# A Fourier filter and an eight-expert layer on one core: zero stores, table loads, casts and the last inverse in another order

## The reference, cut to what matters

```python
def _attn_ref(x, filt_r, filt_i):            # x: 8 x 3072 x 256
    X = np.fft.rfft(x, axis=1)
    Y = X * (filt_r + 1j * filt_i)[None]
    return np.fft.irfft(Y, n=x.shape[1], axis=1)

def _moe_ref(x, w_gate, w1, w2, capacity):   # x: 24576 rows of 256, 8 experts, F = 1024
    N, D = x.shape
    logits = x @ w_gate
    expert_idx = np.argmax(logits, axis=1)
    # gate_w: the softmax probability of the chosen expert
    # rows go to their expert in order of index, at most 768 each; later ones are dropped
    h = np.maximum(np.einsum('ecd,edf->ecf', disp, w1), 0.0)
    y = np.einsum('ecf,efd->ecd', h, w2)
    # out[i] = gate_w[i] * y[expert, place] for kept rows, 0 for all others
```

## Time and profile before

| | us |
|---|---|
| median of 3 runs | 518.39 |
| lowest and highest | 517.58, 519.9 |
| the profiled execution | 520.91 |
| its span in the profile | 519.0 |

### The profile page before, as it was taken

The page is one execution under the profiler, slowest core; times in us unless marked ns, Lnnn a source line. Parts: engine busy times, 40 slices in busy tenths (PEclk is TensorE's granted clock), DMA queues, the critical chain, the costliest instruction groups (busy, mean ns, idle before and its releaser), DMA issues.

```text
span 519.0 us, 12606 instructions
## 1 busy us (share of the span) xinstructions
PE 472.5 (91%) x5432; PEld 428.4 (83%) x5432; DVE 243.5 (47%) x381; ACT 231.8 (45%) x434; POOL 182.2 (35%) x158
## 2 busy tenths in 40 slices
PE   5888999999999786399889999999999999999994
PEld 5767887588875472399889989999999999999993
DVE  1195538893499951478155303334432453134200
ACT  3634566555665465062154523434452454433320
POOL 0000000000000060053457788644877556684222
PEclk9999999999999999599899998999999999999997
DMA  8990000850017599900413159631199320681001
GB/s 291 412 370 7 1 3 3 282 209 3 3 44 228 213 373 378 337 3 21 143 42 121 52 168 403 219 124 53 39 383 357 90 86 32 230 336 45 32 33 35
DMA packets 37169, 80.47 MB, mean 155 GB/s; under 512 B 4944, under 2 KB 13808, under 8 KB 36592
## 3 DMA queue, kind: packets, MB, share of 16 engines
q1 hardware_dynamic: 30832, 66.92, 35.7%
q0 software_dynamic: 6272, 12.65, 7.2%
HBM read 40.20 MB, written 39.35 MB: 153 GB/s over the span
## 4 chain that ended last, share of the span: by engine, by line
PE 76%; issue 5%; DMA 5%; DVE 4%; SPq 4%; POOL 3%; ACT 1%; POOLq 0%; DVEq 0%; ACTq 0%
PE psum L1194 24%; PE psum L1208 22%; PE psum L435 7%; PE psum L422 6%; PE psum L452 4%; PE psum L406 4%; SPq L373 4%; DMA w_raw<-in_w 4%; PE psum L510 3%; PE psum L476 2%; DVE prod L726 2%; PE psum L579 2%; PE psum L466 1%; POOL o_gate L1098 1%; POOL out L1114 1%
## 5 line engine op out<-in xcount | busy, mean ns | idle before, releaser
L1023 DVE SCALAR_TENSOR_TENSOR hl<-psum,hh 128x384 fp32r<-128x384 f32 x128 | 69.7, 556 | 151.1 <-ACT hh L974 151.1
L1208 PE MATMUL psum<-w2h,hh 128*128 128x256 f32 x384 | 110.5, 288 | 0.0
L1208 PE MATMUL psum<-w2l,hh 128*128 128x256 f32 x384 | 109.2, 284 | 0.0
L1208 PE MATMUL psum<-w2h,hl 128*128 128x256 f32 x384 | 109.1, 284 | 0.0
L1194 PE MATMUL psum<-xh,w1h 128*128 128x384 f32 x256 | 87.5, 342 | 15.1 <-DVE xl L764 11.8
L974 ACT ACTIVATE hh<-psum 128x384 fp32r<-128x384 f32 x128 | 61.9, 492 | 75.1 <-PE psum L1194 74.9
L1194 PE MATMUL psum<-xl,w1h 128*128 128x384 f32 x256 | 87.0, 340 | 0.0
L1194 PE MATMUL psum<-xh,w1l 128*128 128x384 f32 x256 | 86.8, 339 | 0.0
L726 DVE TENSOR_TENSOR prod<-psum,fab 128x1024 f32<-128x1024 f32 x48 | 56.5, 1219 | 53.7 <-PE psum L406 42.6
L1114 POOL DMA_INDIRECT out<-o_out,token x48 | 50.6, 1054 | 85.6 <-ACT o_out L983 66.7
L1208 PEld LDWEIGHTS psum<-w2l,hh 128*128 128x128 f32 x384 | 74.3, 194 | 0.0
(11 more groups left out here) (107 smaller groups left out, 596.3 us busy)
## 6 DMA issues: line engine op xcount, KB each, us to landing
out<-zero SPq DMA_DIRECT2D x24, 1024.0 KB, 15.1
w_raw<-in_w SPq DMA_DIRECT2D x14, 1024.0 KB, 5.7
x_in<-in_x SPq DMA_DIRECT2D x18, 512.0 KB, 8.0
y_rows<-y SPq DMA_DIRECT2D x12, 512.0 KB, 4.5
fab<-in_fab SPq DMA_DIRECT2D x4, 1024.0 KB, 13.3
first_raw<-in_w SPq DMA_DIRECT2D x2, 1024.0 KB, 9.2
wbi<-in_wbi SPq DMA_DIRECT2D x4, 384.0 KB, 15.5
y_rows<-y SPq DMA_DIRECT2D x6, 256.0 KB, 9.0
```

The lines of the kernel that those rows point to most:

```text
L1023: nc.vector.scalar_tensor_tensor(out=hl[:, b % 2, f, :], in0=ps[(2, 3, 6, 7)[f % 4]][:, 0:TOK], scalar=0.0, in1=hh[:, b % 2, f, :].bitcast ...
L1208: mm = nc.tensor.matmul(ps[4 + (b * ST + s) % 2][:, 0:D], hx[:, b % 2, f, s * P:(s + 1) * P], wt[k][:, f, :], start=(f == 0 and m == 0), s ...
```

## The change

- The nine zero stores move on SP from the end of `sp_last_stage` to the end of `sp_last`, behind the loads of expert 1 and the row stores.
- At the start, tables 2 and 3 are loaded ahead of the second batch instead of behind it.
- In `pe_stage` the table of the stage's tokens moves in the last group from ahead of the inverse of group 6 to behind it; in the expert part it moves from behind down(0,2) to ahead of it.
- At a stage's end the inverse of group 7 comes ahead of all four turns of the next stage; ScalarE's list follows.
- ScalarE's two casts of expert 0 move one group up, from groups 6 and 7 to 5 and 6.
- VectorE makes expert 1's `w2l` after the route's last steps and the tokens instead of before them.

```diff
@@ sp_last_stage, sp_last
-            if r == 0:
-                sp.wait_ge(zero_set, 1)
-                sp.nop(nofuse=True)
-                for k in range(FIRST_ZEROS):
-                    sp.dma_start(out_z[k], zero_view).then_inc(first_zeroed, 16)

         def sp_last(sp, t, r):
             raw_load(sp, r, 1, 0)
             raw_load(sp, r, 1, 1)
             for c in range(products(t) // 2):
                 y_store(sp, t, c)
+            if r == 0:
+                sp.wait_ge(zero_set, 1)
+                sp.nop(nofuse=True)
+                for k in range(FIRST_ZEROS):
+                    sp.dma_start(out_z[k], zero_view).then_inc(first_zeroed, 16)
@@ pe_stage
-                    if h == NG - 1:
-                        pe_table(pe, tok, 7)
                     for i in turned_at(h):
...
                     if h == RANK_STEP:
                         pe_rank(pe, tok, 7)
+                    if h == NG - 1:
+                        pe_table(pe, tok, 7)
...
-            if a is not None:
-                pe_turn_z(pe, a, 0, r)
-                pe_turn_z(pe, a, 1, r)
             pe_inverse(pe, t, NG - 1)
             if a is not None:
-                pe_turn_z(pe, a, 2, r)
-                pe_turn_z(pe, a, 3, r)
+                for g in range(ZB):
+                    pe_turn_z(pe, a, g, r)
@@ act_stage
+                if t == last - 1 and h == NG - 3:
+                    act_split(act, r, 0, 0)
                 if t == last - 1 and h == NG - 2:
-                    act_split(act, r, 0, 0)
-                if t == last - 1 and h == NG - 1:
                     act.wait_ge(b_done, t * NG + NG - 2)
                     act_split(act, r, 0, 1)
-            if a is not None:
-                act_turned_z(act, a, 0)
-                act_turned_z(act, a, 1)
             act_back(act, t, NG - 1)
             if a is not None:
-                act_turned_z(act, a, 2)
-                act_turned_z(act, a, 3)
+                for g in range(ZB):
+                    act_turned_z(act, a, g)
@@ dve_experts
-                low_split(dve, r, 1, 1)
                 route(HOT, ROUTE_STEPS)
                 both()
+                low_split(dve, r, 1, 1)
                 turned(2)
@@ pe_experts
-            downs(0)
+            down(0, 0)
+            down(0, 1)
             if r == 0:

                 pe.wait_ge(hl_done, 2 * FT)
                 pe_table(pe, last - 1, 7)
+            down(0, 2)
             down(1, 0)
@@ sync, run
-                load_tables(sp, 0)
-                load_tables(sp, 1)
+                for g in range(4):
+                    load_tables(sp, g)
                 for c in range(NCH):
                     x_load(sp, first + 1, c, first)
-                load_tables(sp, 2)
-                load_tables(sp, 3)
```

10 lines of the change are left out of this document (5 added, 5 removed).

## The result

| | kernel before | changed kernel |
|---|---|---|
| median of 4 runs each, side by side on one chip, us | 517.99 | 510.67 |
| lowest and highest | 516.22, 519.9 | 509.57, 511.71 |
| the profiled execution | 520.91 | 511.06 |
| its span | 519.0 | 509.2 |
| TensorE matmuls busy | 472.5 (91%) | 474.1 (93%) |

The ratio is 0.9858, with a 95% interval of 0.9816 to 0.99: 7.3 us faster, where 12.9 were forecast. The predicted 505.5 is 5.2 us too low, and the time lies 0.7 above the upper end of the range, 510.0.

What follows compares the result with a forecast made beforehand. TensorE, 91% busy, was taken as the bound, with its idle stretches and slow clock recoverable. Terms -11.8 - 1.9 + 3.5 - 1.4 - 0.2 - 1.1 = -12.9 us, applied to the 518.39 median, gave 505.5; range 501.5 to 510.

Steps and rivals of the forecast that it cites:

- part 3: Expert part, table ahead of down(0,2) and w2l later: +1.8 to 1.9 us at turn(2) alone, masked while zeros end late.
- part 4: Stage ends, last inverse ahead of the turns hides TensorE's wait for t_in: -0.7 us each, -1.4 in all.
- part 5: End of stage 2, table behind inverse(6) and earlier casts: -0.2 us; stop in the logits gone: -1.1; neither bounded above 0.
- late instruction fetch: Last logits of stage 2: TensorE's 1.16 us stop taken for a fetch that freed DMA engines would spare, -1.1 us.
- GpSimd's chain: From zeros' end at 229.6 through output sends and block 2's gather to turn(2) at 240.8; cost with late zeros +3.5 us.
- no cost taken: Row stores before ScalarE's relu in up(0): landing put at 3 to 4 us within some 4 us of slack, cost 0.
- (a): Zeros end before 228, so the table's order sets turn(2): +1.9 us in place of +3.5, 503.9; chance 0.2.
- (b): Zeros take 31 us or more: +3.4 us more, 508.9; chance 0.12.
- (c): Row stores land late beside the zeros, TensorE stops some 5 us at up(0)'s fifth group: 510.6; chance 0.08.
- (d): Instruction-fetch stalls move under the zeros, beside up(0) and up(1): up to 3.1 us, 508.6; chance 0.04.
- (e): Slower than before: GpSimd's wait for zeros at turn(2) eats the gain, zeros ending from 245: 521; chance 0.03.
- (f): Expert-1 load leaves early but a gather or gate row holds the start: total as before, 518; chance 0.03.

Runs made afterwards that it cites:

- part 1 alone: Kernel before with only the nine zero stores moved behind the row stores: 517.65 against 524.81 us, ratio 0.9849.
- parts 3 and 4 undone: Two kernels, each the changed kernel with one order restored: expert table and w2l, ratio 0.9823; turns ahead of the last inverse, 0.9886.
- part 5 undone: Changed kernel with stage table again ahead of inverse(6) and ScalarE's expert-0 casts a group later, run twice: ratios 0.9862 and 0.9849.
- all together: Changed kernel with zeros one by one, row-store wait late, old expert and stage table orders and cast places, run twice: ratios 0.9711 and 0.9722.
- zeros early with part 3 undone: Changed kernel with zeros in one burst behind the constants and the old order of expert table and w2l: 509.97 us, ratio 0.9799.
- part 6 undone: Changed kernel with the second x again ahead of tables 2 and 3: 517.22 us, ratio 0.9827.
- late-relu experiment: Changed kernel with ScalarE's wait for the row stores moved from the first relu to its first write of o_out: 516.67 us, ratio 0.9842.

## Why the prediction was wrong, step by step

**Right.** The loads leave at 182 (181.7), up(0) waits for nothing and runs at full clock, the two stops of 0.68 go, and so does the one in the last logits. (The prediction has the loads land before 195 at 14.3 us from 183.3; that sum gives 197.6, still ahead of the 199.27 that it needs.) turn(2) follows up(1) by 28.9, within the 28 to 32 named. The zeros bind: in the ten profiles of kernels that have them behind the rows (the changed one three times, and those with one part undone or done alone), turn(2) comes 39.3 to 40.1 us after the first zero's issue, whatever stands between, although up(1) moves against the zeros by 2 us. In the kernels without zeros there it is up(1) that sets it, 27.6 to 28.0 us later with the table ahead of down(0,2) and 26.0 to 26.3 with the old order. The masking of part 3 and its price alone (1.4 to 2.0 measured, 1.8 to 1.9 forecast) are thereby shown. So is what part 4 gives at the stage ends (0.8 and 0.8 measured, 0.7 each forecast).

**Mis-sized, up to up(2).** The sum gave -12.9 there; the two profiles have -10.1 (258.93 to 248.81). The constant just named splits the difference of 2.8, since only two terms lead to turn(2) when the zeros bind.

**When the zeros start: 203.6, not 202.0, 1.6 late.** The step that failed is part 5, its "-0.2" and "-1.1" with nothing above 0 as the worst case. TensorE's rank matmuls start only 1.4 us earlier than before (202.72 against 204.13), not 2.7; the last 0.3 is SP, which has to issue the last rows first. At the last forward step of stage 2 TensorE is still 2.5 us ahead (173.12 against 175.58), more than part 4's 1.4: part 4 gave 1.7, and 0.8 is luck, since the stops at 33 and 40 us happened to be shorter. From there to the rank matmuls the changed kernel takes 29.60 us and the kernel before 28.55. So this stretch, where part 5 was to gain 1.3, lost 1.05. The 1.41 for `hot_hi` went, but a stop of 1.17 us came up inside the table instead, 0.85 ahead of inverse(7), and half clock behind them:

```profile
175.84 0.30 PE L533 MATMUL psum<-hot_hi,hot_lo 128*128 128x96 bf16 x3
177.31 1.05 PE L533 MATMUL psum<-hot_hi,hot_lo 128*128 128x96 bf16 x21 [1.17 <-issue]
179.22 2.39 PE L422 MATMUL psum<-wbi,prod 64*64 64x96 f32 x64 [0.85 <-DVE prod L728]
182.57 4.76 PE L466 MATMUL psum<-v_in,wgs 128*32 128x128 f32 x96 [0.96 <-ACT v_in L623]
```

The same stretch, from the start of the last forward step of stage 2 to that of the rank matmuls, in all eighteen profiles:

| us | profiles |
|---|---|
| 26.84, 26.85 | zeros early, zeros one by one |
| 28.55 | kernel before |
| 28.75 to 28.82 | part 1 alone; parts 3 and 4 undone; part 5 undone, first; zeros left out; all together, both times |
| 29.59, 29.60 | changed kernel, first two; zeros early with part 3 undone |
| 30.28 | changed kernel, third |
| 32.45 to 34.51 | kernel before once more; part 5 undone, second; part 6 undone; row-store wait moved |

In all sixteen profiles with the zeros moved the stop of 1.16 us is gone from the logits, so that much of "moving zeros also frees the DMA engines around 185 us" came. But in most of them the time is lost again some microseconds later, in a stop in the last turns or in half clock. The table's place itself is worth 0.14 us where no half clock follows (logits to logits 51.99 against 52.13). Part 5 as a whole shows in no median: 518.63 undone against 517.79.

The stop in the table is not the stop of the earlier trace rows moved. It stands after the same 3 matmuls of the table in all eleven profiles with part 5's order, and that of the earlier trace rows after the same 42 logits in both profiles of the kernel before. In the list of the changed kernel these two places are 21 + 64 + 42 = 127 matmuls apart. The two early stops, at 33 to 35 and at 39 to 41 us, are 127 matmuls apart as well, at the same places in all eighteen profiles. With a weight load for each matmul that makes 254 instructions, near the 256 that the prediction cites for a block. So the prediction's late instruction fetch is well supported, though no row shows a fetch. In the old order the wait of 1.41 us for `hot_hi` stands some 2 us ahead of the earlier of the two places, and no stop shows there. That this wait hides it fits, and is not shown. Whether the stop needs full DMA engines is open too. The share is 0.18 in the stretch of the stop itself (columns as above), but they had been nearly full until 176:

```profile
176.00:177.30 1.30, 0.14 (x3) 0.04 (x1) 1.30 (x2) 0.84 (x2) 0.00 (x0) 1.00 0.18 56
```

The Trainium skill ("Runtime: NRT & Kernel Launch", Instruction fetch mechanics) calls such fetches mostly hidden; here stops of 0.2 to 2.4 us without any semaphore stand in every profile, two of them always at the same places, so the trace agrees only in part.

**The zeros' length and GpSimd's chain: 40.0 us from the first issue to turn(2), not 38.8.** The zeros took 29.1 us at 356 GB/s in all, not 27.6 at 360. At 356 GB/s, 29.1 us are 10.4 MB, and the sum had 9.9: the rate costs 0.3 and the bytes 1.2. The likeliest source of the 0.4 MB more is the load of expert 2's w1, issued right behind the zeros at 221.98; no run took it away, so this stays open. GpSimd's chain is 10.9, not 11.2.

**Wrong, but without effect.** The row stores were put at "no cost taken", and up(0) does stop at its fifth group (0.71 us), which the prediction had named as a sign of being wrong. They cost 2.1 us between up(0) and up(1) (11.49 against 9.35 with the row-store wait moved; the forecast had 9.1), more than half of it ahead of up(1), which the prediction did not see: the late relu delays VectorE's low halves, behind which `xl` of block 1 is made, at 213.53 to 214.54. The estimate of 3 to 4 us for landing was right (3.6 to 4.6); what was wrong was the slack. The last rows are ready at 202.37, but SP needs until 203.51 to issue their last two stores. ScalarE's four delayed relus come in one row of 1.64 us, and the low half then comes another 0.6 us later. The late-relu experiment shows the cost and that it is hidden, since the zeros bind: 2.1 us gained at up(1), none at turn(2).

**Wrong: from the profiled execution to the median.** The profiles differ by 9.8 us and the medians by 7.3. The prediction took its sum against one execution of 520.91 and carried it over by difference. But that execution lies above its median by 2.5 to 2.9, that of the changed kernel by 0.4. Where its excess lies is known only in part. Between the two profiles the clock does not account for the difference. Added up by stretches of a microsecond, the granted clock lacks 10.2 us of full speed ahead of the last 10 us in the profile of before and 6.8 in that of after, but 5.0 of the 10.2 fall between 206 and 216.5 us, where TensorE stands idle, as in this stretch (columns as above):

```profile
210.00:211.00 1.00, 0.00 (x0) 0.00 (x0) 0.00 (x0) 0.00 (x0) 0.00 (x0) 0.50 1.00 331
```

While TensorE worked, the half clock cost 5.2 us before and 6.8 after. The two early stops, 3.1 us together in the earlier trace rows, are the longest of all eighteen profiles, where they go from 1.0 to 3.1; the changed kernel's has 1.8. That may be 1.3 of it. Against its own kind this execution may well be one of low clock, 0.975: on the chip with the second measurement the kernel before took 519.3 to 522.1 us at a mean clock of 0.972 to 0.976 and 515.8 to 517.9 at 0.980 to 0.982. Which of its rows are the longer for it is open. Put against medians, the forecast should have been smaller by what this one execution had in excess. The other two measurements of the same pair give 10.2 and 8.5 us, so the 7.3 is also at the low end of what the change is worth: the mean of the three is 8.7 us, 1.7%.

So of the 5.2 us by which the forecast missed, 2.8 (1.6 and 1.2) lie in the two terms up to up(2), 0.3 in the rest of the span (260.07 before, 260.39 after), and 2.1 in the step from execution to median.

**The rivals.** (a) did not happen with the zeros behind the rows, and the runs with the zeros elsewhere show its mechanism, at +1.4 to +2.0. (b) is the nearest: the zeros took 29.1, between 27.6 and 31. (c) has the right wait with the wrong cause and size. (d) did not come: no stop stands under the zeros but the 1.25 us ahead of up(1), and although its row says "issue", it went with the late relu. (e) and (f) are excluded. The range was too narrow at the top because part 5 was given no way to lose, and the choice of execution no width at all.

## What to carry to other kernels

A transfer that is moved off one critical wait must be priced at the next wait for it, here GpSimd's 14.5 us. Taking that wait away gained nothing by itself between up(0) and turn(2), since two others (the table's place, the late relu) lay right behind it. With it gone, mending those two took 5 us off this way. The stores cost nothing where the DMA engines were idle, one at a time; in one burst they delayed TensorE's first stages by some 3 us. An order that is measured as harmless while another wait is longer (the table, the relu) has to be measured again when that wait is gone. Before a sum is put against a median, compare the profiled execution's time and clock with the other runs, and forecast from a typical one. Half clock while an engine stands idle costs nothing and does not belong in such a sum.

## What the runs showed of the hardware

- **Half clock comes in pieces.** The granted clock falls to half in stretches that each cost a busy TensorE 1.7 us (in the changed kernel 244 to 248 and 302 to 307 us, and two such on end from 179 to 187). One program has another number of them from execution to execution, and the times of the changed kernel on one chip follow: 507.11 and 507.22 us at a mean clock of 0.992, 509.02 at 0.988, 513.04 and 513.58 at 0.982. This spread of 6 us is larger than most parts of the change. The stretch where the profiles differ most is the end of stage 2: 28.55 and 32.74 us in the two of the kernel before, 29.59 to 30.28 in the three of the changed one.
- **Some stops without a semaphore sit at fixed places of the instruction list.** In all eighteen profiles two stand 127 matmuls apart, at 33 to 35 us (0.2 to 0.95 us long) and at 39 to 41 us (0.5 to 2.4 us). Their length differs between executions of one program (1.31, 1.31 and 1.86 us in the changed kernel at the second place), and a new order of the program decides whether a wait stands ahead of such a place or not.
- **A store of 256 KB to HBM takes 3 us and more to land.** 3.3 us at the median in the changed kernel, 3.0 to 3.4 for the early ones of the six, at a DMA share of 0.57, and 4.1 for the last. With a load of 1 MB right behind them instead of the zeros the last took 5.0 us in two profiles (zeros left out, zeros one by one) and 3.8 in a third (all together). The Trainium skill ("DMA: Bandwidth & Descriptors", Anatomy of one DMA), for DMAs that GpSimd issues, puts most of a transfer's fixed cost on the confirmation from the target memory; these are SP's, and the runs show the delay, not its cause.
